# Dividing the first constant transfers by columns and moving the first pair's loads between the bias steps' stores

## What is computed

```python
# q, k, v: (4, 8, 576, 64); w1: (1, 32), b1: (32,), w2: (32, 8)
rel    = pos[:, None] - pos[None, :]
x      = log1p(abs(rel)) / log1p(max(pos, 1))[:, None]    # 576 x 576
h      = maximum(x[..., None] * w1 + b1, 0)               # 32 hidden units
bias   = h @ w2                                           # 576 x 576 x 8 heads
attn   = softmax(q @ k.T / 8 + bias) @ v                  # 4 batches, 8 heads
# then: 8 experts, one per token, out = p[e] * (relu(x @ w1[e]) @ w2[e])
```

## Time and profile before

| what | value |
|---|---|
| median of 3 runs | 714.79 us (714.54 to 715.71) |
| the profiled execution's own time | 715.85 us |
| its span in the trace | 714.1 us |
| mean granted TensorE clock | 0.971 |
| bias loop in the span | about 8.0 to 66.0 us |
| attention | about 66 to 376 us |
| routing and experts | about 376 to 714 us |

### The profile page before, as it was taken

How to read it: one execution, slowest core, us unless ns; L and a number is a source line. 1 busy time by engine, 2 the same in 40 slices (tenths; PEclk the granted TensorE clock), 3 DMA queues, 4 the chain that set the end, 5 groups by cost and what they waited for, 6 DMA issues and landing times. The chain is left out here.

```text
span 714.1 us, 14144 instructions
## 1 busy us (share of the span) xinstructions
PE 658.3 (92%) x4353; PEld 528.3 (74%) x4353; DVE 376.8 (53%) x803; ACT 343.8 (48%) x727; POOL 194.1 (27%) x178
## 2 busy tenths in 40 slices
PE   6777899999999999999955899999999999999994
PEld 3224788888888888888735788888888888888883
DVE  5999565555555555556657642478424422122220
ACT  4997566666666666666530341466424422212221
POOL 4000614444444444445501011112111111111101
PEclk9999999999999999999975899999999999999998
DMA  7778534447444444444074941148310011111100
GB/s 166 202 195 206 109 68 100 99 97 212 98 100 96 99 97 98 98 101 94 18 264 151 344 152 64 45 154 308 104 44 31 35 44 44 44 44 44 44 0 1
DMA packets 67960, 77.05 MB, mean 108 GB/s; under 512 B 46543, under 2 KB 47055, under 8 KB 67920
## 3 DMA queue, kind: packets, MB, share of 16 engines
q1 hardware_dynamic: 63392, 64.58, 34.4%
q0 software_dynamic: 4144, 11.54, 5.1%
q10 hardware_dynamic: 384, 0.44, 0.2%
HBM read 69.06 MB, written 11.27 MB: 112 GB/s over the span
## 5 line engine op out<-in xcount | busy, mean ns | idle before, releaser
L790 DVE CUSTOM_DVE_ANT_0 sm<-ps_s,bias 128x576 f32<-128x576 f32 x128 | 91.7, 754 | 66.9 <-PE ps_s L1075 66.8
L610 ACT ACTIVATE sm<-sm,negmax 128x576 f32<-128x576 f32 x144 | 111.9, 778 | 5.7 <-DVE negmax L790 5.6
L1250 PE MATMUL ps_pv<-w2hi,hThi 128*128 128x512 f32 x200 | 80.5, 402 | 1.4 <-DVEq L979 1.4
L999 DVE TENSOR_TENSOR hTlo<-ps_s,hThi 128x512 fp32r<-128x512 f32 x50 | 32.2, 686 | 92.8 <-ACT hThi L724 92.6
L1250 PE MATMUL ps_pv<-w2hi,hTlo 128*128 128x512 f32 x200 | 78.3, 391 | 0.0
L1250 PE MATMUL ps_pv<-w2lo,hThi 128*128 128x512 f32 x200 | 77.9, 390 | 0.0
L1146 PE MATMUL ps_pv<-pT,vt 128*64 128x320 f32 (+1 forms) x512 | 69.1, 410 | 4.5 <-issue 0.7
L506 POOL CAST ksplit<-raw 128x1152 fp32r<-128x1152 f32 x15 | 17.2, 1147 | 195.8 <-DMA raw<-in_kq_dram 195.7
L1227 PE MATMUL ps_s<-w1hi,xThi 128*128 128x512 f32 x200 | 64.9, 406 | 4.9 <-DVE xTlo L971 3.1
L716 ACT ACTIVATE hsb<-ps_s 128x512 f32<-128x512 f32 x25 | 15.0, 599 | 110.6 <-PE ps_s L1227 104.6
L558 POOL DMA_INDIRECT out_dram<-ysb,sidx x25 | 25.5, 1020 | 156.5 <-ACT ysb L731 156.5
(11 more groups left out here) (184 smaller groups left out, 1293.0 us busy)
## 6 DMA issues: line engine op xcount, KB each, us to landing
w1raw<-in_moe_w_dram SPq DMA_DIRECT2D x18, 1024.0 KB
w2raw<-in_moe_w_dram SPq DMA_DIRECT2D x18, 1024.0 KB
raw<-in_kq_dram SPq DMA_DIRECT2D x32, 432.0 KB, 5.1
bias<-stage SPq DMA_DIRECT2D x32, 288.0 KB, 3.2
raw<-in_kq_dram SPq DMA_DIRECT2D x32, 128.0 KB, 4.9
vt<-in_v_dram SPq DMA_DIRECT2D x32, 128.0 KB, 2.4
tokens_dram<-xl SPq DMA_DIRECT2D x64, 64.0 KB, 1.7
bias_tail<-stage SPq DMA_DIRECT2D x4, 144.0 KB, 2.4
```

Source lines behind the costliest of these rows:

```text
L610: nc.scalar.activation(probs, probs, ACT.Exp, scale=-1.0, bias=negmax[:, u % 2, hd:hd + 1], accum_out=sums[:, pr % 2, 2 * t + hd:2 * t + h ...
L790: nc.vector.tensor_tensor_reduce(sm[:, u % 2, S * hd:S * (hd + 1)].rearrange("p (a c) -> p a c", a=2), ps_s[:, hd, :, 0:HALF], bias.rearra ...
L999: V.tensor_tensor(hTlo[:, 4 * i:4 * i + 4, :].rearrange("p k t -> p (k t)"), ps_s[:, 1, i, :], hThi[:, 4 * i:4 * i + 4, :].bitcast(F32).re ...
L1250: last = nc.tensor.matmul(ps_pv[:], h[:, f, :], w[:, f, :], start=f == 0 and h is hThi and w is w2hi, stop=f == KF - 1 and h is hTlo)
```

## The change

- `load_window` gets a part: part 0 is columns up to `WNEAR = S + D = 640` of the window, part 1 the rest (640 to 1152). `load_slopes` is new and divides `rps` the same way: part 0 is the columns from `CNEAR = 128` to 140, part 1 the columns 0 to 127. The semaphore `consts_in` becomes `near_in` for parts 0 and `far_in` for parts 1.
- SyncE issues near windows and slopes of groups 0 and 1, the four loads of `w2bd`, then the far windows of groups 0 and 1 and the far slopes of all four groups. ScalarE issues the near parts of groups 2 and 3 and then two far windows.
- VectorE waits for the near parts alone and makes the near part of `slope` (52 elements a partition instead of 564). After its tiles of step 2 it waits for the far parts, makes the other 512 elements and waits for its own result. ScalarE waits for that before its tile of step 4.
- The first pair's loads leave the opening. After the store of each even step from 2 on, SyncE issues one piece: steps 2 to 12 one part of `raw` each, 14 and 16 half of `vt` each (two DMAs), 18 and 20 one load of the gates each.
- TensorE does three identity products instead of four ahead of the steps.

```diff
+WNEAR = S + D
+CNEAR = P * FULL // G
...
-        def load_window(queue, g):
-
-            rows = slice(C * g, C * (g + 1))
-            queue.dma_start(win[rows, (G - 1) * g:LT], ltab[rows, 0:LT - (G - 1) * g]).then_inc(consts_in, 16)
-            queue.dma_start(rps[rows, :, 0:NCOL - G + 1],
-                            bass.AP(tensor=rpsi.tensor, offset=g,
-                                    ap=[[NCOL, C], [C * NCOL, G], [1, NCOL - G + 1]])).then_inc(consts_in, 16)
+        def load_window(queue, g, part):
+
+            rows, lo, hi = slice(C * g, C * (g + 1)), ((G - 1) * g, WNEAR)[part], (WNEAR, LT)[part]
+            queue.dma_start(win[rows, lo:hi], ltab[rows, lo - (G - 1) * g:hi - (G - 1) * g]).then_inc((near_in, far_in)[part], 16)
+
+        def load_slopes(queue, g, part):
+            rows, lo, hi = slice(C * g, C * (g + 1)), (CNEAR, 0)[part], (NCOL - G + 1, CNEAR)[part]
+            queue.dma_start(rps[rows, :, lo:hi],
+                            bass.AP(tensor=rpsi.tensor, offset=g + lo,
+                                    ap=[[NCOL, C], [C * NCOL, G], [1, hi - lo]])).then_inc((near_in, far_in)[part], 16)
...
             for g in range(2):
-                load_window(nc.sync, g)
+                load_window(nc.sync, g, 0)
+                load_slopes(nc.sync, g, 0)
             sp.wait_ge(zeroed, 1)
             for g in range(G):
                 nc.sync.dma_start(w2bd[C * g:C * (g + 1), H * g:H * (g + 1)], w2).then_inc(w2_in, 16)
+            for g in range(2):
+                load_window(nc.sync, g, 1)
+            for g in range(G):
+                load_slopes(nc.sync, g, 1)
...
+            def load_first_pair(i):
+
+                if i < 2 * PARTS:
+                    load_qk_part(0, i // PARTS, i % PARTS)
+                elif i < 2 * PARTS + 2:
+                    sp.wait_ge(zeroed, 10)
+                    load_v_half(0, i - 2 * PARTS)
+                elif i < 2 * PARTS + 4:
+                    load_gates(i - 2 * PARTS - 2)
...
-            load_qk(0)
-            sp.wait_ge(zeroed, 10)
-            load_v(0)
-            for half in range(2):
-                load_gates(half)
             for m in range(STEPS):
...
+                if m >= 2 and m % 2 == 0:
+                    load_first_pair((m - 2) // 2)
...
             for g in range(2, G):
-                load_window(nc.scalar, g)
+                load_window(nc.scalar, g, 0)
+                load_slopes(nc.scalar, g, 0)
+            for g in range(2, G):
+                load_window(nc.scalar, g, 1)
             act.wait_ge(bias_prep, 2)
...
+                if m == SLOTS:
+                    act.wait_ge(bias_prep, 3)
...
-            dve.wait_ge(consts_in, CONSTS)
+            dve.wait_ge(near_in, CONSTS)
             dve.wait_ge(w1_small, 32)
-            nc.vector.tensor_scalar(slope[:, :, 0:NCOL - G + 1], rps[:, :, 0:NCOL - G + 1], w1s[:, 0:1], None, ALU.mult).then_inc(bias_prep, 1)
+            nc.vector.tensor_scalar(slope[:, :, CNEAR:NCOL - G + 1], rps[:, :, CNEAR:NCOL - G + 1], w1s[:, 0:1], None,
+                                    ALU.mult).then_inc(bias_prep, 1)
...
+                if m == SLOTS - 2:
+                    dve.wait_ge(far_in, CONSTS)
+                    nc.vector.tensor_scalar(slope[:, :, 0:CNEAR], rps[:, :, 0:CNEAR], w1s[:, 0:1], None,
+                                            ALU.mult).then_inc(bias_prep, 1)
+                    dve.wait_ge(bias_prep, 3)
...
-            ident_products(4)
+            ident_products(3)
```

More of the change, by code:

```diff
@@ L200, in build @@
         ps_x = psum("ps_x", [P, BANK])
-        consts_in = sem("consts_in")
+        near_in = sem("near_in")
+        far_in = sem("far_in")
         turn_in = sem("turn_in")
```

## The result

| | kernel before | changed kernel |
|---|---|---|
| median of 6 runs | 715.25 us | 717.30 us |
| lowest and highest | 714.27 to 717.28 | 715.72 to 718.62 |
| ratio | | 1.0035, 95% interval 1.0019 to 1.0050 |
| profiled execution | 715.85 us, span 714.1 | 715.72 us, span 714.0 |
| VectorE's first tile | 8.03 us | 6.34 us |

The changed kernel is 0.35% slower, 2.05 us between the medians. It won 2.5 us before step 3 and lost 4.2 us after it. The end of the step loop does show it, and it is the number that I use to tell the kernels apart: in seven kernels with several runs, median time less loop end is 651.0 to 652.6 us, though each loop end is read from one execution.

A forecast was written before the change was run, and what follows sets the result against it. VectorE sets the rhythm from step 3, so shifts there move the kernel's end one for one. 2.2 us won at the start less 1.1 lost to loads gives 1.1: 714.79 to 713.7 us, range 712.0 to 715.7.

The forecast's parts named there:

- The start: Opening up to VectorE's step 3: first tile at 6.18, 1.85 us earlier; step 3 at 11.69, 2.2 us gained.
- full clock through 14 us: TensorE's steps 0 to 3: granted clock stays at 1.00; gain 2.2 us, against 1.7 with the half clock.
- the wait for the far parts: VectorE after step 2, at 11.2: nothing charged for waiting on these loads; bound 1.0 us.
- The near slopes: VectorE before its first tile: 52 elements instead of 564 shrink the instruction from 0.52 us to 0.15 to 0.2.
- case 2: Rival: loads hide, queue at 268 GB/s or more; 712.6 us, or 711.7 with constants in by 4.7; chance 0.27.
- the loads between the stores: SyncE's queue, steps 2 to 20: 1.49 MB among stores stall the copies to `stage`; 1.1 us lost.
- The rate: Queue with loads and stores mixed: 243 GB/s, so one big part of `raw` takes 1.8 us.
- The room: Time a store may land late before delaying a copy to `stage`: 0.8 us early, 2.2 us later.
- The clock: TensorE's granted clock in steps 0 to 3: expected full; a half clock would cut the gain from 2.2 to 1.7 us.
- ScalarE's slack: ScalarE's copies to `stage`: stalls up to about 0.4 us cost nothing, so 0.4 was subtracted from the 1.5 us sum.
- Case 4: Rival: every copy to `stage` waits on a store behind a load, queue about 205 GB/s; 717.2 us; chance 0.10.
- the row of 229 GB/s: Profile rate of the queue crowded with stores alone; at it the loads would lose 1.9 us instead of 1.1.

The follow-up runs named there:

- loads_behind_loop: Changed kernel, with the first pair's loads issued behind the last store instead of between the stores; 724.6 us in one run.
- division_alone: Constants divided as in the changed kernel, first pair's loads issued at the start behind the far parts; ratio 1.0026 to the kernel before.
- the later-pieces run: Changed kernel with the same ten pieces after every second store from step 14 to 32 instead of 2 to 20; 715.5 us in one run.
- the kernel with GpSimd's queue: Changed kernel with the first pair's loads issued by GpSimd on its own queue, SyncE having only stores; 717.1 us in one run.
- loads_between_alone: Kernel before, constants undivided, only the first pair's loads moved between the stores; ratio 1.0066, median 720.77 us.

## Why the prediction was wrong

I forecast 713.7 us, 712.0 to 715.7. The median is 717.3, outside the range and on the other side.

**The start was right.** First tile 6.34 (forecast 6.18), TensorE 8.13 (8.34), full clock through 14 us, step 3 at 11.37 (11.69), the wait for the far parts free. `b1s` landed 3.0 us after its issue, at 5.17, and `w2bd` after 2.3 to 2.5; what ended VectorE's wait was `rps`, at 5.42. With fewer bytes ahead of them these landings came 1.4 and 1.7 us sooner after their issue than the earlier trace rows. The near slopes missed: 0.58 us for 52 elements where I had 0.15 to 0.2. That the first tile still fits is partly luck, a landing 0.3 us earlier and slopes 0.4 us longer. The gain was 2.5 us against 2.2.

The 0.58 us are not the work of 52 elements. Changed kernel, then the same instruction in `loads_behind_loop` and in `division_alone`:

```profile
5.75 0.20 POOL L495 MEMSET fold<- 128x128 f32 x1
```

```profile
5.19 0.81 DVE L783 TENSOR_SCALAR slope<-rps,w1s 128x52 f32<-128x52 f32 x1 [3.42 <-DMA rps<-in_rpsi_dram]
```

```profile
5.54 0.46 DVE L783 TENSOR_SCALAR slope<-rps,w1s 128x52 f32<-128x52 f32 x1 [3.77 <-DMA rps<-in_rpsi_dram]
```

In all ten kernels with divided constants this instruction began at 5.19 to 5.54 and ended at 5.97 to 6.00, within 0.05 us of the end of GpSimd's fourth memset in a row. So its end hangs on GpSimd, as far as rows can tell (no run moved the memsets), and then no earlier landing would have moved the first tile, and the 711.7 us that case 2 had for one were out of reach.

**The step that failed is "the loads between the stores".** It gave 1.1 us lost; 4.2 were. Two of its terms, the rate and the room, were mis-sized, and a third, the clock's price for the stall, was not in it.

1. The rate. I took 243 GB/s from one 4 us stretch, with the DMA engines busy for 0.94 of it. The full, mixed queue moved 201 to 231 (214 in the first 6 us, 219 to 228 in the later-pieces run). I let the big part delay the stores by 1.8 less 0.3 us; step 3's last store, issued 1.9 us behind it, landed 2.6 us later than its fellows.
2. The room. I used 0.8 us, from the stores of later steps. The stall came at step 3's three tail stores, issued last at 17.91 for a copy due at 20.4: 2.5 us allowed, 2.0 needed, 0.5 of room. I had written that SyncE was late there and that one more issue goes in, and put neither into the sum. The landing of 4.6 us less those 2.5 is the measured stall of 2.17; I had 0.7.
3. The clock. I asked whether the start would keep it and never whether the stall that I forecast would cost it. The clock fell within TensorE's pause of 2.32 us and stayed at half from 23.6 to 27, and VectorE lost 2.91 us for ScalarE's 2.17. In the kernel with GpSimd's queue ScalarE waited 1.36 us at 20.54, the clock stayed at 1.00, and VectorE lost 1.14. The difference (0.7 more than the wait, against 0.2 less) puts the clock's share near 1 us; `loads_between_alone` has the same 0.7 more (2.94 for 2.2). In `division_alone`, also with the clock at half, VectorE lost 3.90 us in two breaks for ScalarE's 3.70, which by the same reckoning puts it near 0.4. So the share is an estimate of 0.4 to 1 us, and no run isolated it.

The later waits (0.96, 0.40 and two short ones) were forecast as 0.8 at step 13 and cost VectorE 1.25. In sum, 2.91 us for 0.7, 1.25 for 0.8, and the 0.4 of ScalarE's slack that I had taken off are the 3.1 us between 1.1 and 4.2.

**The rival that came true.** Case 4, with a chance of 0.10, had the queue at 205 GB/s, 4.6 us of stalls and 717.2 us. It was right in its mechanism and nearly in its size; that every copy would wait was not so, five did. That its 717.2 lies beside the measured 717.3 is partly luck: it had 2.4 us between the kernels, the medians have 2.05, and the kernel before came out at 715.25 this time, not 714.79. Its chance was too low because I set aside the row of 229 GB/s, stores alone and in line, for the one higher row that had loads in it. At 229 my own sum gave 1.9 us lost and 714.5; with the room of 0.5 (0.3 more) and the clock's 0.4 to 1 us it comes to 2.6 to 3.2, still under the 4.2 measured.

**Why the profiled span hides it.** Loop end is 1.71 us later than before, the end of the span 0.1 us earlier. The time comes back at places that the change doesn't touch. One of them, kernel before and then changed kernel:

```profile
86.00:88.00 2.00, 2.00 (x11) 1.98 (x11) 1.92 (x6) 0.13 (x1) 1.92 (x2) 0.50 0.00 0
```

```profile
86.00:88.00 2.00, 1.75 (x14) 1.75 (x15) 0.93 (x3) 0.52 (x2) 1.94 (x3) 1.00 0.00 0
```

In the execution before, the clock was at half there; in this execution of the changed kernel it had been at half at 72 to 74 instead, and the delay shrank from 1.7 to about 0.5 us by 100 us. The rest went in the routing, where the clock also fell later. In the six runs the mean granted clock was 0.973 where the span was 714.0 to 715.0 and 0.970 where it was 716.2 to 716.9. How much each of these places gave back is not shown by one execution of each kernel. So one profile's end says little about a change of 2 us here; the loop end and the medians do.

**Two figures that were weighed.** The mixed queue moved 201 to 231 GB/s. The Trainium skill's 436 GB/s ("DMA: Bandwidth & Descriptors", Anatomy of one DMA), which I had set aside, is far from that; the page fits it for a DMA that GpSimd issues, and these are SyncE's. The near slopes, in pieces of 52 bytes, landed after 2.0 to 2.7 us, the windows of 79 to 80 KB beside them after 2.0 to 2.6; the loss that the Trainium skill states for pieces below 512 bytes (same page, Specifications) is not seen on so few bytes.

## What to carry to other kernels

Moving transfers out of an opening is only free if the queue has spare rate where they go: add their bytes to what the loop asks for and compare with a crowded stretch of the same queue, not with its best one. Measure the room of the very stores that stand behind them, including how late their issuer runs, and ask of every forecast stall whether TensorE's clock survives it. Then look for the stretch where the queue is idle: here two issues into the 2.5 us in which SyncE waited, with the small parts moved to later steps, turned 0.35% slower into 0.24% faster. Where a wait names an engine, check when that engine's work had ended; a DMA may stand behind it.

## What the hardware showed that I had not expected

- Loads issued from another engine's queue delay the stores as much as loads in the same one: 4.5 us of waits against 4.3.
- A GpSimd elementwise instruction of 1.79 us stretched VectorE's tiles beside it from 0.56 to 0.87 and 0.97 us, and cost more than the 0.48 us that the same work takes on VectorE.
- VectorE's near slopes (52 elements a partition) took 0.46 to 0.81 us and ended at 5.97 to 6.00 us in all ten kernels that have them, within 0.05 us of the end of GpSimd's memsets, whenever they began. The 564 elements of the kernel before, at 7.18 and clear of those memsets, took 0.52 us.
- Tiny loads issued by GpSimd landed 2.7 and 3.0 us after issue with few bytes ahead of them, and 3.9 and 4.4 with the full constants in the queues.
